# Warm-up of TensorE in 96 short matmuls instead of 12 long ones, and the last tile's copy in three pieces instead of two

## What is computed

```python
# 1: linear attention with a decaying state; batch 4, heads 8, seq 768, head_dim 64
state = gamma * state + outer(k_t, v_t);  y_t = scale * (q_t @ state)
# 2: dense layer, 512 -> 2048 -> 512
h = x @ w_in;  r = maximum(h, 0);  x2 = (s * (r * r) + b) @ w_out
# 3: eight experts, 512 -> 1024 -> 512, each takes exactly 3072 / 8 = 384 tokens
logits = x2 @ w_gate      # tokens are given out greedily by descending logit
out[mask] = maximum(x2[mask] @ w1[e], 0) @ w2[e]
```

## Time and profile before

| what | value |
|---|---|
| median of 3 runs | 930.32 us |
| the three runs | 928.18, 930.32, 930.51 us |
| the profiled execution's own time | 928.14 us |
| its span (first to last instruction) | 926.3 us |
| PE busy | 919.4 us, 99% |
| DVE, ACT, POOL busy | 516.3, 295.9, 225.4 us |
| device memory read and written | 128.54 and 63.18 MB |

### The profile page before, as it was taken

One profiled execution on the slowest core, in us unless ns is written; L12 is line 12 of the kernel. 1 busy time (PEld: TensorE's weight loads), 2 busy tenths in 40 slices (PEclk: granted clock), 3 DMA queues, 4 the chain that ended last, 5 costly groups with the idle time before them and its releaser, 6 DMA issues.

```text
span 926.3 us, 18516 instructions
## 1 busy us (share of the span) xinstructions
PE 919.4 (99%) x7449; PEld 749.2 (81%) x7449; DVE 516.3 (56%) x1218; ACT 295.9 (32%) x557; POOL 225.4 (24%) x216
## 2 busy tenths in 40 slices
PE   8999999999999999999999999999999999999998
PEld 6777877777877777777777777778998998998997
DVE  6775666555655466467676765773534434434420
ACT  3543344434444352010101010101443534534521
POOL 5232322222221000001110111001443553553621
PEclk9999999999999999999999999999999999999999
DMA  9986666656764478667676767284635635635500
GB/s 334 334 312 238 252 244 218 239 210 236 262 229 182 182 250 326 241 208 226 215 237 195 241 208 229 82 267 152 232 117 180 204 119 178 204 121 175 182 35 34
DMA packets 81317, 192.93 MB, mean 208 GB/s; under 512 B 8880, under 2 KB 17584, under 8 KB 81232
## 3 DMA queue, kind: packets, MB, share of 16 engines
q1 hardware_dynamic: 77200, 178.98, 57.0%
q0 software_dynamic: 3840, 12.59, 4.1%
q10 hardware_dynamic: 192, 0.19, 0.1%
HBM read 128.54 MB, written 63.18 MB: 207 GB/s over the span
## 4 chain that ended last, share of the span: by engine, by line
PE 99%; DVE 1%; issue 0%; POOLq 0%; POOL 0%; ACT 0%; DVEq 0%
PE bank L1203 29%; PE bank L1086 29%; PE bank L1247 14%; PE bank L1262 14%; PE bank L1011 2%; PE bank L921 1%; PE bank L879 1%; PE bank L909 1%; PE bank L1223 1%; PE bank L945 1%; PE bank L1116 1%; PE bank L884 0%; PE bank L970 0%; PE bank L981 0%; PE bank L1035 0%
## 5 line engine op out<-in xcount | busy, mean ns | idle before, releaser
L1086 PE MATMUL bank<-x,wi_hi 128*128 128x512 f32 x768 | 240.0, 394 | 0.0
L1086 PEld LDWEIGHTS bank<-x,wi_hi 128*128 128x128 f32 x768 | 141.9, 188 | 36.8 <-ACT u_sb L745 5.9
L700 POOL TENSOR_TENSOR w_lo<-w_raw,w_hi 128x512 fp32r<-128x512 f32 x72 | 93.4, 1306 | 299.9 <-ACT w_hi L818 299.8
L1086 PE MATMUL bank<-x,wi_lo 128*128 128x512 f32 x384 | 149.4, 390 | 0.0
L1333 DVE SCALAR_TENSOR_TENSOR u_sb<-u_sb,cst 128x512 f32<-128x512 f32 x96 | 80.5, 838 | 102.6 <-ACT u_sb L745 102.6
L1203 PE MATMUL bank<-wo_b,g_back 128*128 128x512 f32 x552 | 136.9, 398 | 0.0
L818 ACT ACTIVATE w_hi<-w_raw 128x512 fp32r<-128x512 f32 x128 | 76.6, 636 | 155.0 <-DMA w_raw<-in_w 154.5
L1203 PEld LDWEIGHTS bank<-wo_b,g_back 128*128 128x128 f32 x552 | 100.0, 188 | 19.2 <-issue 0.8
L745 ACT ACTIVATE u_sb<-bank 128x512 f32<-128x512 f32 x96 | 57.4, 598 | 180.7 <-PE bank L1086 144.0
L1640 DVE TENSOR_TENSOR w_lo<-w_raw,w_hi 128x512 fp32r<-128x512 f32 x56 | 60.1, 1073 | 63.1 <-ACT w_hi L818 62.6
L1635 DVE SCALAR_TENSOR_TENSOR e_lo<-bank,e_hi 128x384 fp32r<-128x384 f32 x64 | 35.4, 554 | 100.4 <-ACT e_hi L856 100.4
(11 more groups left out here) (209 smaller groups left out, 1210.5 us busy)
## 6 DMA issues: line engine op xcount, KB each, us to landing
g_rows<-g_sb SPq DMA_DIRECT2D x96, 512.0 KB, 3.1
g_back<-g_rows SPq DMA_DIRECT2D x80, 512.0 KB, 4.0
w_raw<-in_w SPq DMA_DIRECT2D x128, 256.0 KB, 3.7
x_rows<-x SPq DMA_DIRECT2D x25, 256.0 KB, 4.7
g_back<-g_rows SPq DMA_DIRECT2D x16, 384.0 KB, 4.6
kT<-in_k_turned SPq DMA_DIRECT2D x22, 256.0 KB, 4.4
qT<-in_q_turned SPq DMA_DIRECT2D x22, 256.0 KB, 4.7
vin<-in_v SPq DMA_DIRECT2D x22, 256.0 KB, 3.8
```

What stands on the lines that cost most here:

```text
L700: pool.tensor_tensor(low, w_raw[:, (p * E_PIECES + n) % RAW, :], high.bitcast(F32), ALU.subtract).then_inc(w1_lo_done, 1)
L1086: last = pe.matmul(up[i % 2][:, :], w[:, t, fs], x[:, half, t, :], start=(n_ == 0), stop=(n_ == len(products) - 1))
```

## The change

The number of `keep_busy` matmuls goes from 5, 2 and 5 to 40, 16 and 40, and each streams 64 columns instead of 512. The last tile is copied in one quarter (128 columns), another quarter, and the second half; the added semaphore `late_quarter_copied` guards the second quarter in PE's stream and in SP's.

```diff
-FIRST_IDLE, MIDDLE_IDLE, SECOND_IDLE = 5, 2, 5
+FIRST_IDLE, MIDDLE_IDLE, SECOND_IDLE = 40, 16, 40
+IDLE_COLS = 64
...
+        late_quarter_copied = sem("late_quarter_copied")
...
             def store_row(tile):
                 sp.wait_ge(x2_copied, tile + 1)
                 if tile == LATE:
+                    sp.wait_ge(late_quarter_copied, 1)
                     sp.wait_ge(late_half_copied, 1)
...
-                cols = slice(0, DM // 2 if tile == LATE else DM)
+                cols = slice(0, P if tile == LATE else DM)
                 act.activation(x2[:, tile % OUT_STAGE, cols], out_bank(tile)[:, cols], ACT.Copy).then_inc(x2_copied, 1)
                 if tile == LATE:
+                    act.activation(x2[:, tile % OUT_STAGE, P:DM // 2], out_bank(tile)[:, P:DM // 2], ACT.Copy).then_inc(late_quarter_copied, 1)
                     act.activation(x2[:, tile % OUT_STAGE, DM // 2:], out_bank(tile)[:, DM // 2:], ACT.Copy).then_inc(late_half_copied, 1)
...
             def keep_busy(n, free):
 
                 for _ in range(n):
-                    pe.matmul(by_pair(free[:, :]), ones16[:, :], ones16[:, :].unsqueeze(1).to_broadcast([P, 4, P]), start=True, stop=True)
+                    pe.matmul(free[:, 0:IDLE_COLS], ones16[:, :], ones16[:, 0:IDLE_COLS], start=True, stop=True)
...
             for t in range(DT):
                 if t == 0:
                     pe.wait_ge(x2_copied, TILES)
+                elif t == 1:
+                    pe.wait_ge(late_quarter_copied, 1)
                 elif t == DT // 2:
                     pe.wait_ge(late_half_copied, 1)
```

## The result

The changed kernel is slower: 931.72 us median of 13 runs (929.88 to 934.95) against 928.33 us for the kernel before in 13 runs (927.56 to 930.51). The ratio is 1.0035, 95% interval 1.0023 to 1.0047. Its runs also spread more, over 5.1 us against 3.0. The profiled execution took 929.99 us (span 928.2), 1.85 us more than the one of before; that is half of the median's difference, so one trace alone can't explain the whole.

What follows compares the result with a forecast made beforehand. PE, busy 99% of the span, was taken to bound the kernel. Profiled: 928.14 - 0.87 + 0.6 - 0.1 = 927.8 us; with the median's 2.2 us on top 929.9 us, no change (0.80), range 927.1 to 932.0.

Steps and rivals of the forecast that it cites:

- The columns, the three groups: Warm-up: pairs of 64 columns take 0.053, later 0.029 us; first and second group add zero, middle 0.47 instead of 0.43 us.
- The hole at 17.6 us: PE's wait for code in L964: the code now comes in time, hole gone, -0.87 us (bounds -0.87 and 0).
- A new hole in L879: PE waits for the second code block near 19 to 20 us: 0 to 1.6 us, taken as 0.6.
- Last tile: Copy in three pieces lets PE's L1215 start earlier: -0.1 us (bounds -0.11 and +0.1).
- The next boundary: Second code boundary moves from the dense stage at about 27 us into the L879 loop of 19.88 us.
- the DMA side: DMA traffic gains two thirds of one 16 KB packet beside 192 MB: zero.
- (b): Both holes in full or pairs paced by their loads: +0.6, at most +1.7 us, median 930.9 to 932.0; chance 0.13.
- (c): Slower: short matmuls warm the clock less, start at half pace for longer, up to +12.3 us, 942 us; chance 0.10.
- The level: Median of the shown runs lies 2.2 us above the profiled execution; the same distance was added to the forecast.
- (d): Faster: runs at 930.3 and 930.5 us come from a warm-up or code wait now removed; median 927.1; chance 0.10.

Runs made afterwards that it cites:

- after_pad72: The changed kernel with 72 more instructions (increments of an unused semaphore) in the dense stage: 930.89 us, ratio 1.0024 to the kernel before.
- warm_only: The kernel before with only the short warm-up, the last tile's copy left as it was: 931.74 us, ratio 1.0032.
- after_late88: The changed kernel with 88 semaphore increments added from the matmul at 59 us on: 931.42 us, ratio 1.0045 to the kernel before.
- before_pad168: The kernel before with 168 more instructions (unused semaphore increments), one ahead of each dense matmul from 21 us on: 930.44 us, ratio 1.0022.
- before_pad240: The kernel before with 240 more instructions (unused semaphore increments) over the first 40 us of the dense stage: 932.54 us, ratio 1.0043.
- before_turned8: The kernel before with the fourth load of w_out turned (1 MB) issued at step 8 instead of 9: 928.25 us, ratio 0.9999.

## Why the prediction was wrong

**The columns, the three groups:** right. 0.053 and 0.029 us a pair as taken, no delay from the first group, 0.1 us at `apply(0)` where I had nothing. The trace's record of full speed begins at 4.1 to 7.4 us in eight traces with the long warm-up and at 4.2 to 7.1 in seven with the short one, so the 96 short matmuls show no weaker warming. The Trainium skill's figure of 62 ns a matmul with hardware decode off ("TensorE: Matmul & The Clock Gate", part 1) set no bound here: the trace has 29 ns. Whether decode was on or off no run shows.

**The hole at 17.6 us goes:** right; the code packet came at 9.4 us instead of 16.1, and neither trace of after has a hole in L964. The hole's own size was overrated as a saving, though: of the eight traces with the old warm-up four have it (0.9 to 1.3 us) and four don't, although all run the same program up to 21 us. So it is in some executions of before only.

**A new hole in L879 of 0 to 1.6 us:** right in place, and in size but for one trace. It was 0 in the trace of after and of after_pad72, 0.6 to 1.8 us in the other five with the short warm-up.

**Last tile, -0.1 us:** right to the hundredth: 1.35 to 1.24 us.

**The step that failed** is "The next boundary, 128 pairs on, moves from the dense stage at about 27 us to the old pair 260". I moved two boundaries of 59 and stopped, since behind 21 us PE is filled and I took a filled stretch as a safe one. The windows of after show what it is made of:

```profile
53.30:56.20 2.90, 2.90 (x144) 1.00 0.79 309
56.20:57.66 1.46, 0.16 (x1) 1.00 0.94 328
```

Where an attention chunk is woven in, 144 pairs pass in 2.9 us, more than a whole block of code. Counted in recorded instructions, the block ahead was entered at 53.3 us; the packet went at 55.3 and PE ran on at 57.7: 4.4 us, the last 2.4 of which lie behind the packet's start, as 2.2 to 2.8 did at every hole. A block that is used up in some 3 us leaves no room for that, unless its successor was asked for before. A purely dense one, at 0.23 us a matmul (57.66 to 57.89 above), lasts 29 us.

A short block alone is not enough, though. Before has a block of 3.2 us between 51.2 and 54.4 us, with DMA as full, and after has one of 1.9 us between 105.1 and 106.9, both without a hole. The windows of the last us ahead of each block and of the block itself, first before:

```profile
50.21:51.21 1.00, 1.00 (x6) 1.00 1.01 395
51.21:54.42 3.21, 3.21 (x125) 1.00 1.05 415
```

then after, at the hole and at the block without one:

```profile
52.32:53.32 1.00, 1.00 (x39) 1.00 1.01 408
53.32:56.36 3.04, 3.04 (x144) 1.00 0.75 293
104.06:105.06 1.00, 1.00 (x7) 1.00 0.03 12
105.06:106.93 1.87, 1.87 (x129) 1.00 0.40 156
```

The blocks without a hole were entered out of long matmuls, 6 or 7 in the last us, and their successor's packet started 1.4 and 3.0 us ahead of the entry. The block with the hole was entered out of short ones, 39 in that us, and the packet started 1.9 us behind the entry. Over the 16 traces 52 blocks of 1.9 to 3.3 us went by without a hole, every one with the packet started at least 0.1 us ahead of the entry; at all 23 holes it started 1.5 to 6.4 us behind it. So the fetch isn't tied to the moment at which the recorded stream enters a block, as I had taken it: it came earlier where the matmuls ahead of the block were long. Why, no run shows.

Adding 168 instructions moved a block's start from 51.2 us, among long matmuls, to 53.3, inside the chunk; the term that I had at 0 was 1.2 to 2.5 us. The clock's fall that warm_only's trace shows came after the other hole, that of L879. Over the executions, though, falls go with the hole at 57.7 us: 14 of 36 of the changed kernel, `warm_only` and `after_late88` have one, none of 27 of the three changed kernels padded from 21 us on. Whether that hole or something else between 21 and 59 us brings them stays open.

**The wait for `early_qT`** wasn't in the forecast: I held the DMA side at zero because one packet of 16 KB is nothing beside 192 MB. It moved from 16 to between 9 and 11 us, in front of a load that PE was waiting for; whether it held that load back was not taken apart.

**Rivals:** (b), both holes in full, was nearest with 930.9 to 932.0 and got 0.13; its second hole lay elsewhere, and its sum took the first hole as gone (-0.87), against its name. (c) named the clock, with another cause: the warm-up's weakness was not the point, a fall after a hole was. **The level** was wrong as well: I added the 2.2 us by which the median of three runs lay over the profiled execution. Over 13 runs the median is 928.33, 0.2 us above it, and the two runs at 930 us on which (d) rested were spread. That 931.72 us falls inside the range of 927.1 to 932.0 is luck: against before I allowed at most +1.7 us and it was +3.4, and the level, 2 us too high, made up for it.

The Trainium skill ("Runtime: NRT & Kernel Launch", instruction fetch mechanics) says that a 16 KiB boundary is mostly hidden. The traces agree with "mostly": of some 60 packets none to four leave a hole. These, and the clock's falls that go with them, are the greater part of this change's effect; what share each has in the 3.4 us isn't shown.

## What to carry to other kernels

Adding or removing instructions, even free ones, shifts every later block of code on that engine; where a block is entered and used up within a burst of short instructions, faster than the next can come, the engine stands still. Before judging a small change by its local cost, run it again with some free instructions added: if the ratio swings by as much as the change did, the position may be all that was measured. When a block must come in a tight place, keep large loads out of the DMA queues just ahead of it.

## What the runs showed of the hardware

- PE's code came in packets of 16.4 KB, one for every 128 pairs or so. A share of 25.6% of 16 engines over 0.25 us, in the row above, is 1.0 us of one engine for one packet. It shares the DMA engines with data: it comes late behind queued data (shown by moving one load), and data probably comes late behind it. For the second there is only a pattern: in the five short-warm-up traces where PE reached `scores(2)` early enough to need it, `early_qT` was waited for by 1.0 to 1.2 us with the code packet at 9.4 to 10.6 us; with the packet at 13.9 us or later the wait was at most 0.2. No experiment took it apart.
- The granted clock fell to half for 3.4 us 0.7 to 1.5 us behind the end of a hole with 1.8 to 2.1 us of idle PE in three traces (warm_only, before_pad168, before_pad240). In the traces it did not fall after holes of 1.5 us and less, nor after the one of 2.5 us at 62 us of warm_only, which came right out of and into dense matmuls, while the three came out of short ones. What decides between them stays open.
- A late rise of the clock was absorbed by the wait for code: before_turned8, with full speed from 7.4 us on, ran `scores(0)` to 1.2 us behind before, but had no hole in L964, was 0.1 us behind from there on and had the same span of 926.3 us.
